# Fused attention and feed-forwards on one Trainium2 core: sums and reciprocals four units ahead, four score buffers, GpSimd's subtractions at later units

## The reference

```python
scores = scale * q @ k^T - slope[head] * dist      # keep: first n_global keys, and the last n_local before the row
a = exp(scores - max); a = a / (sum(a) + 1e-9)
x = (a @ v)  as 1536 tokens x 512
h = x @ w_in                                       # 512 -> 2048
g = (a0 + a1 h + a2 h^2 + a3 h^3) / (1 + |b0||h| + |b1| h^2 + 1e-6)
x = g @ w_out                                      # 2048 -> 512
h = x @ w2_in; s = h * softmax(h); y = layer_norm(s) * g_ln; out = y @ w2_out   # 512 -> 1024 -> 512
```

## Time and profile before

| what | value |
|---|---|
| time, median of 3 runs (lowest to highest) | 487.11 us (486.02 to 490.15) |
| the profiled execution's own time | 483.23 us |
| its span in the profile | 481.2 us |
| PE / DVE / ACT / POOL busy | 469.0 / 377.9 / 271.3 / 55.8 us |
| TensorE's granted clock | 1.0 in all forty slices |

### The profile page before, as it was taken

How to read it: one execution, slowest core, us unless ns; L and a number is a source line. 1 busy time by engine, 2 the same in 40 slices (tenths; PEclk the granted TensorE clock), 3 DMA queues, 4 the chain that set the end, 5 groups by cost and what they waited for, 6 DMA issues and landing times.

```text
span 481.2 us, 7546 instructions
## 1 busy us (share of the span) xinstructions
PE 469.0 (97%) x2734; PEld 383.1 (80%) x2734; DVE 377.9 (79%) x705; ACT 271.3 (56%) x481; POOL 55.8 (12%) x123
## 2 busy tenths in 40 slices
PE   7889999999999999999999999999999999999997
PEld 5667778888888878888888788888888888888885
DVE  6989989999999989877889999999685555555550
ACT  6989998656656465455555545543454333333341
POOL 4868770000000000000000000000000000000000
PEclk9999999999999999999999999999999999999999
DMA  8897964000000000000033445331012222222201
GB/s 296 295 384 268 350 252 178 1 0 1 0 1 1 0 1 0 1 1 0 1 93 105 131 140 158 113 93 44 1 44 67 66 65 65 65 68 78 72 23 44
DMA packets 25665, 42.91 MB, mean 89 GB/s; under 512 B 2080, under 2 KB 16800, under 8 KB 24480
## 3 DMA queue, kind: packets, MB, share of 16 engines
q1 hardware_dynamic: 23760, 36.64, 22.2%
q0 software_dynamic: 1296, 5.24, 3.7%
q10 hardware_dynamic: 576, 0.60, 0.4%
HBM read 33.04 MB, written 3.15 MB: 75 GB/s over the span
## 4 chain that ended last, share of the span: by engine, by line
PE 85%; ACT 7%; DMA 3%; DVE 3%; POOL 1%; issue 1%; SPq 0%; ACTq 0%; DVEq 0%
PE ps L1198 9%; PE ps L1199 9%; PE ps L1200 9%; PE ps L1129 8%; PE ps L1130 8%; PE ps L1131 8%; ACT probs L481 5%; PE ps L1263 5%; PE ps L1261 5%; PE ps L1218 5%; PE ps L1262 5%; PE ps L1217 5%; PE ps L1216 5%; PE ps L1244 2%; DMA bank_a_raw<-in_w_in 2%; PE ps L1095 2%
## 5 line engine op out<-in xcount | busy, mean ns | idle before, releaser
L1198 PE MATMUL ps<-gate_hi,bank_b_hi 128*128 128x512 f32 x192 | 74.9, 390 | 0.5 <-DVE tok_lo L942 0.5
L1129 PE MATMUL ps<-tok_hi,bank_a_hi 128*128 128x512 f32 x192 | 75.1, 391 | 0.0
L1130 PE MATMUL ps<-tok_lo,bank_a_hi 128*128 128x512 f32 x192 | 74.7, 389 | 0.0
L1199 PE MATMUL ps<-gate_lo,bank_b_hi 128*128 128x512 f32 x192 | 74.7, 389 | 0.0
L1131 PE MATMUL ps<-tok_hi,bank_a_lo 128*128 128x512 f32 x192 | 74.7, 389 | 0.0
L1200 PE MATMUL ps<-gate_hi,bank_b_lo 128*128 128x512 f32 x192 | 74.7, 389 | 0.0
L543 ACT ACTIVATE quad<-ps 128x1024 f32<-128x1024 f32 x23 | 23.7, 1030 | 57.8 <-DVE rest L880 57.8
L481 ACT ACTIVATE probs<-negs,small 128x256 f32<-128x256 f32 (+1 forms) x96 | 46.0, 484 | 0.8 <-DVE small L726 0.7
L442 POOL TENSOR_SCALAR probs<-probs,small 128x256 f32<-128x256 f32 (+1 forms) x96 | 42.6, 465 | 15.4 <-DVE small L737 15.4
L862 DVE SCALAR_TENSOR_TENSOR quad<-quad,small,absh 128x1024 f32<-128x1024 f32 x23 | 29.5, 1281 | 18.0 <-ACT absh L546 17.8
L1198 PEld LDWEIGHTS ps<-gate_hi,bank_b_hi 128*128 128x128 f32 x192 | 36.0, 188 | 8.7 <-issue 1.2
(11 more groups left out here) (103 smaller groups left out, 948.1 us busy)
## 6 DMA issues: line engine op xcount, KB each, us to landing
v_sb<-in_v_win SPq DMA_DIRECT2D x8, 704.0 KB, 6.6
bank_a_raw<-in_w_in SPq DMA_DIRECT2D x4, 1024.0 KB, 9.0
bank_b_raw<-in_w_out SPq DMA_DIRECT2D x4, 1024.0 KB, 7.1
stage_hi<-tok_hi SPq DMA_DIRECT2D x12, 256.0 KB, 2.7
stage_lo<-tok_lo SPq DMA_DIRECT2D x12, 256.0 KB, 2.8
out_dram<-out_sb SPq DMA_DIRECT2D x12, 256.0 KB, 2.0
q_sb<-in_q_t SPq DMA_DIRECT2D x14, 192.0 KB, 5.1
k_sb<-in_k_win SPq DMA_DIRECT2D x7, 384.0 KB, 8.2
```

Source lines behind the costliest of these rows:

```text
L1129: pe.matmul(banks(bank, 1), bank_a_hi[:, f, ws], x_hi, start=(k == 0), stop=False)
L1130: pe.matmul(banks(bank, 1), bank_a_hi[:, f, ws], x_lo, start=False, stop=False)
L1198: pe.matmul(banks(4 + k, 1), bank_b_hi[:, f, ws], g_hi, start=first, stop=False)
L1199: pe.matmul(banks(4 + k, 1), bank_b_hi[:, f, ws], g_lo, start=False, stop=False)
```

## The change

It does four things. `SUMS_AHEAD` goes from 2 to 4, and the sums and reciprocals move within DVE's step: from the head of the step to the place behind the copy, around the first shift of unit n+7. The prologue of the loop makes the sums of units 2 and 3 as well. `negs` and `negmax` get four buffers in place of two, so a shift waits for the exponentials of unit n-4; the new buffers lie in a free gap of the work area and in the last columns of `tok_hi` and `tok_lo`, which are written only after the last exponential. POOL's cast goes from unit 8 to unit 7, and its four subtractions from units 15, 21, 27, 33 to units 21, 23, 33, 35.

```diff
     PB, TB = 8, 4
-    negs = [[at(f"negs{i}{h}", [P, WIN], F32, w + (2 * i + h) * KB) for h in range(2)] for i in range(2)]
+    NB_NEGS = 4
+    own_negs = 4 * (KT * T - (S // 2) - WIN)
+    negs_at = [w + j * KB for j in range(4)] + [w + (20 + j) * KB for j in range(2)] + [TOK_HI + own_negs, TOK_LO + own_negs]
+    negs = [[at(f"negs{i}{h}", [P, WIN], F32, negs_at[2 * i + h]) for h in range(2)] for i in range(NB_NEGS)]
...
-    negmax = [cols(2) for _ in range(2)]
+    negmax = [cols(2) for _ in range(NB_NEGS)]
...
-    AHEAD, SCORES_AHEAD, SUMS_AHEAD = 6, 8, 2
+    AHEAD, SCORES_AHEAD, SUMS_AHEAD = 6, 8, 4
...
-    POOL_IN, SPLIT_FROM, SPLIT_EVERY = 4, 15, 6
-    LOADS_AT, CAST_AT = (1, 3, 4, 5), 8
+    POOL_IN, SPLITS_AT = 4, (21, 23, 33, 35)
+    LOADS_AT, CAST_AT = (1, 3, 4, 5), 7
...
                 if n == CAST_AT:
                     cast_w_in()
-                f, part = divmod(n - SPLIT_FROM, SPLIT_EVERY)
-                if part == 0 and 0 <= f < POOL_IN:
-                    split_in_low(f)
+                if n in SPLITS_AT:
+                    split_in_low(SPLITS_AT.index(n))
...
         def attend_shift(n, h):
 
-            par, i = n % 2, n % BLOCKS
+            buf, i = n % NB_NEGS, n % BLOCKS
...
-            if h == 0 and n >= 2:
-                dve.wait_ge(exp_ready, 2 * (n - 1))
+            if h == 0 and n >= NB_NEGS:
+                dve.wait_ge(exp_ready, 2 * (n - NB_NEGS + 1))
...
         def attend_pair(n):
...
-            if n + SUMS_AHEAD < HEADS:
-                attend_sums(n + SUMS_AHEAD)
             if k < HEADS:
...
-            if n + SUMS_AHEAD < HEADS:
-                attend_reciprocals(n + SUMS_AHEAD)
...
+            if n + SUMS_AHEAD < HEADS:
+                attend_sums(n + SUMS_AHEAD)
             if k < HEADS:
-                for h in range(2):
-                    attend_shift(k + 1, h)
+                attend_shift(k + 1, 0)
+            if n + SUMS_AHEAD < HEADS:
+                attend_reciprocals(n + SUMS_AHEAD)
+            if k < HEADS:
+                attend_shift(k + 1, 1)
...
             for n in range(2, AHEAD):
                 attend_shift(n, 0)
-                if n == 3:
-                    attend_sums(0)
+                if n % 2:
+                    attend_sums(n - 3)
                 attend_shift(n, 1)
-                if n == 3:
-                    attend_reciprocals(0)
+                if n % 2:
+                    attend_reciprocals(n - 3)
```

More of the change, by code:

```diff
@@ L480, in attend_exp @@
             j = par * 2 + h
-            act.activation(probs[pbuf][:, h, lo:WIN], negs[par][h][:, lo:WIN], ACT.Exp, scale=-1.0,
-                           bias=negmax[par][:, h:h + 1], accum_out=psums[n // 2 % (PB // 2)][:, j:j + 1]).then_inc(exp_ready, 1)
+            act.activation(probs[pbuf][:, h, lo:WIN], negs[n % NB_NEGS][h][:, lo:WIN], ACT.Exp, scale=-1.0,
+                           bias=negmax[n % NB_NEGS][:, h:h + 1], accum_out=psums[n // 2 % (PB // 2)][:, j:j + 1]).then_inc(exp_ready, 1)
         def attend_copy(n):
@@ L721, in attend_shift @@
             lo = 0 if i else P
-            if h == 0 and n >= 2:
-                dve.wait_ge(exp_ready, 2 * (n - 1))
+            if h == 0 and n >= NB_NEGS:
+                dve.wait_ge(exp_ready, 2 * (n - NB_NEGS + 1))
             src = scores_of(n, h)[:, lo:WIN]
             bs = bias[h][:, 0:WIN] if i else bias[h][:, WIN:NB]
-            dve.tensor_tensor_reduce(negs[par][h][:, lo:WIN], src, bs, -SCALE, 3.0e38, ALU.add, ALU.min,
-                                     negmax[par][:, h:h + 1]).then_inc(shifted_ready, 1)
+            dve.tensor_tensor_reduce(negs[buf][h][:, lo:WIN], src, bs, -SCALE, 3.0e38, ALU.add, ALU.min,
+                                     negmax[buf][:, h:h + 1]).then_inc(shifted_ready, 1)
         def attend_sums(n):
```

## The result

| | before | after |
|---|---|---|
| median of the runs compared (lowest to highest, runs) | 486.56 us (484.33 to 490.15, 6) | 480.81 us (480.54 to 482.43, 6) |
| ratio, with its 95% interval | 1 | 0.9884 [0.9856, 0.9912] |
| the profiled execution's own time / its span | 483.23 / 481.2 us | 480.80 / 479.0 us |
| PE's first `up` in the profile | 70.43 us | 68.17 us |

The change makes the kernel 1.2% faster. The forecast was 484.8, within a range of 482.3 to 488.0, with 0.92 on "within 1%". So the size was wrong, the median lies under the range, and "within 1%" did not hold, while the profiled execution came out as the sum said: 480.9 was worked out for it, 480.80 measured. The runs differ by 5.75 us and the two profiles by 2.43. The experiments look for the other 3.3.

A forecast was written before the change was run, and what follows sets the result against it. Attention was taken as bound by ACT, then PE's matmuls decide; the hole's -2.13 and the buffers' -0.16, all else 0, gave -2.3 us: 480.9 for the profiled execution, 484.8 on the median, range 482.3 to 488.0.

The forecast's parts named there:

- What bounds, and the chain of waits: Attention: ACT's list bounds; POOL's subtraction waits 2.79 us for `w_in`, holding multiplications, PE's transposes and ACT's copy.
- The signs: Changed profile: last exponential near 65.3, `up` near 68.1, no POOL transfer wait, PE without idle time from 75 to 165.
- The subtractions, -2.13 and nothing late next: POOL: first subtraction moved behind unit 21, reached at 34.7 at the earliest, after the 31.25 landing, so no wait: -2.13 us.
- The reciprocals cover the doublets: DVE's reciprocals 1.0 us earlier cover the 0.5 POOL lacks behind each subtraction doublet: 0 us, between 0 and +1.0.
- The step's sum: ACT's two units, about 2.6 us against POOL's 3.12 with a subtraction, leave POOL 0.5 behind per step, a doublet 1.0.
- The sums' new wait, 0: DVE: sums of n+4 and n+5 wait for n+5's last exponential, as n+7's shift did before; hidden, 0 us.
- the four buffers, -0.16: They free a step's first shifts and win small ACT holes behind new bias tables: -0.16 us, between 0 and -0.5.
- The cast, 0: POOL's cast issued about 17.2 in place of 20.05; hardly any q, k or v waits on it: 0 us.
- the same difference on the median: The profiled execution's 3.88 us below the median carried over unchanged: 487.11 - 2.3 = 484.8 us.
- the hole: ACT's timeline: late copy after the exponential at 32.74 and late exponential after it, 1.55 + 0.58 = 2.13 us.
- The third rival: Transfers bind again: the first quarter of `w_in` or v's load lands too late, perhaps 1 us given back, 485.8; chance 0.08.
- 1.35 us to spare: Load of v for the next heads lands at 28.8, PE needs it at 30.19; the tightest of all loads.

The follow-up runs named there:

- E3: Kernel before with the first quarter of `w_in` loaded one turn earlier and the cast at unit 7: 480.89 us, ratio 0.9882.
- E10: Kernel before with the first quarter of `w_in` loaded one turn later: 491.53 us, ratio 1.01.
- E8: Kernel before with the moved subtractions and the cast at unit 7, but two buffers and sums two ahead: 482.31 us, ratio 0.992.
- E6: Kernel before with four `negs` buffers alone: 485.07 us, ratio 0.9982.
- E7: Kernel before with only the sums and reciprocals four units ahead at their new place: 485.08 us, ratio 0.9983.
- E12: Kernel after with two `negs` buffers in place of four: 481.98 us, ratio 0.9882.
- E1: Kernel before with POOL's four subtractions alone moved to units 21, 23, 33, 35: 482.57 us, ratio 0.9914.
- E5: Kernel before with only the cast moved to unit 7: 483.78 us, ratio 0.995.
- E4: Kernel before, unchanged, run again for a second profile: 485.85 us, ratio 0.9986.
- E13: Kernel before with 8 added unused identity products on TensorE ahead of unit 16's transposes: 485.80 us, ratio 0.9998.
- E15: Kernel before with the first `w_in` load one turn later and 28 added unused identity products ahead of unit 16's transposes: 491.62 us, ratio 1.01.
- E16: Kernel before with the first `w_in` load one turn later, run a second time: 491.52 us, ratio 1.0105.
- E2: Kernel after with the four subtractions put back behind units 15, 21, 27, 33: 482.35 us, ratio 0.991.
- E9: Kernel before with 18 added unused identity products on TensorE ahead of unit 16's transposes: 485.75 us, ratio 0.9974.
- E11: Kernel after with the first quarter of `w_in` loaded one turn later: 482.02 us, ratio 0.9883.
- E14: Kernel after with the first quarter of `w_in` loaded one turn earlier as well: 480.79 us, ratio 0.9887.

## Why the prediction was wrong, point by point

- **What bounds, and the chain of waits: right.** A wait for a transfer in POOL's queue held multiplications, transposes and copies. E3 removes that wait with an earlier load and cast and gets the whole gain; E10 lengthens it and loses 5 us. The signs held in the profile: the last exponential at 65.31 (65.3 forecast), `up` at 68.17 (68.1), PE busy for all 90.00 us from 75 to 165. That `up` agrees to 0.1 us is partly luck, since the slow start alone can shift it by 1.
- **The subtractions, -2.13 and nothing late next: right for that execution.** The subtraction was forecast for 34.7 at the earliest and came at 35.52, without a wait.
- **The reciprocals cover the doublets: right.** Uncovered they cost some 0.8 us (E8), near the end of the range "0 to +1.0"; covered, ACT has no bracket behind them. The step's sum has a slip: its terms give 2.7 us for ACT's two units and not 2.6, so a doublet leaves POOL 0.8 behind and 0.4 short, which is 0.8 for both. In a step with the subtraction into `tok_lo` the reciprocals start 1.02 us after the copy (53.23 to 54.25) in place of 2.17, 1.15 earlier for a forecast of 1.0.
- **The sums' new wait, 0, and the four buffers, -0.16: not contradicted, but not measured.** E6 and E7 can't tell either from no change, and their intervals are far wider than 0.16. E12's two lowest runs say the same of the buffers.
- **The cast, 0: wrong as a part, harmless in the sum.** Alone it is worth 0.5% [0.3, 0.7], and in that run's profile the quarter of `w_in` lands earlier, the cast being done sooner. The prediction priced only whom the cast might hurt. With the subtractions moved, that gain has no wait left to shorten (E8 against E1: 0.992 and 0.9914). The rule of the Trainium skill on turns between queues (DMA: Bandwidth & Descriptors, "Queues, rings and completion order") goes with that: a cast that flies earlier takes its share earlier. The two landing times of E5 and E4, 9.1 and 10.9 us, agree in direction.
- **The failed step: "the same difference on the median".** It took 2.13 us, the hole in one execution, for the hole of every run. That execution lay 3.88 us under the median, and the text gave that gap but never asked where it lay. E4's profile shows it: 1.12 us more wait, and 1.17 of slower work at half clock after it, counted at `up`. A change that takes the wait away takes all of this, the usual case and not the short one. Worked that way, the time after is the profiled execution less the hole, 480.9, for the median too, since nothing variable is left in it.
- **The range** allowed a stray median, not a variable term in the sum. The third rival's place (transfers) was the right one, with the sign turned round: the transfer bound more in the kernel before. There PE had to wait for v too in some executions (0.43 us in E6's profile, 0.18 in E13's), the load that the prediction gave 1.35 us to spare.
- **The clock** was read as 1.0 in forty slices and given no term. In the usual execution it is not. In E10's profile it fell while PE stood idle, and in E4's after idle time. The Trainium skill (TensorE: Matmul & The Clock Gate, "What's actually happening") says that TensorE's clock steps down after idle time, and these two traces agree. The prediction weighed no such price on PE's 2.06 us, and in that one profile there was none.

So of 5.75 us on the median, 2.4 were the difference as profiled, nearly all of it the hole. The rest is a wait usually longer than in that profile and, in most executions, a half clock after it. How it divides between these two on the median is not measured; in E4 they were about even, and so they are by the estimate above.

## What to carry to other kernels

Set the profiled execution's own time beside the median of the runs before you carry a difference over. If it lies well below and a transfer is waited for on the path, the missing microseconds probably sit in that wait and in what follows it, and a second profile tells. A wait for a transfer costs most in the queue of an engine that others wait for: give it slack by a later use or by an earlier load, one of the two is enough, and expect a narrower spread as well as a lower median.

## What the runs showed of the hardware

- TensorE's granted clock fell to half at a stretch of idle time of 2.12 us (E7), 2.99 (E4), 3.28 behind products (E15), 3.43 (E6), 7.97 (E16) and 8.00 (E10), and did not fall at 2.06, 1.31 (E5), 1.15 (E13) or 0.68 (E2). In E7, E10 and E16 it fell while TensorE still stood; in E4, E6 and E15 it fell 2.3, 1.1 and 0.9 us after TensorE had started again. It stayed at half for some 3.4 us in E4, E6 and E15, 6.8 in E7 and 10.2 in E10 and E16. E8's profile has one more such fall, from 13.2 to 16.6 us, right behind 1.07 us of idle time, where E4's has 1.09 us at the same place and stays at 1.0. So the length of the last idle time alone does not set it. What does is open.
- The first 1024 KB of `w_in`, loaded at the same step in each, took from issue to landing 8.1 (E12), 8.5 (E2), 9.1 (E5), 9.1 (E8) and 9.7 us (after) with the cast at unit 7, and 9.9 (E7), 9.9 (E9), 10.0, 10.9 (E4), 11.2 (E1), 11.6 (E13) and 11.8 us (E6) with the cast at unit 8. The two ranges do not overlap, though only 0.2 us lie between them, and the spread of the second, 1.9 us, is the wait's variable part.
- The profiles of E9, E11, E12 and E14 show a start that is some 1.2 us longer: 24 of PE's first score products of 64x256 stand in one row of 4.5 to 4.8 us, and the next eight start at 12.17 to 12.38, in place of 10.74 to 11.21 in most others (11.67 in E1). In E9, E12 and E14 the granted clock is 1.0 there, in E11 it is at half from 7.2 us on, so the cause is open.
